# Attention and the w3 product in one block of instructions, and the last stretch's width taken by a branch

## What is computed

```python
attn = softmax(where(block_i >= block_j, q @ k.T / 8, -1e9)) @ v        # 4 x 8 heads, 576 x 64
x = attn, heads side by side                                             # 2304 x 512
h = (x @ w1) * (x @ w2) @ w3 ;  x = h @ w_out                             # w3 1024 x 1024, w_out 1024 x 512
noisy = x @ w_gate + log1p(exp(x @ w_noise)) * noise                      # top 2 of 8, softmax weights
out[t] = sum over its 2 experts of weight * relu(x[t] @ e_w1[e]) @ e_w2[e]
```

## Time and profile before

| | us |
|---|---|
| median of 3 runs | 1051.24 (1050.34 to 1051.44) |
| the profiled execution's own time | 1052.73 |
| its span | 1050.6 |
| PE busy | 1019.5 (97%) |
| DVE, ACT, POOL busy | 443.0, 365.1, 540.7 |

### The profile page before, as it was taken

One profiled execution on the slowest core, in us unless ns is written; L12 is line 12 of the kernel. 1 busy time (PEld: TensorE's weight loads), 2 busy tenths in 40 slices (PEclk: granted clock), 3 DMA queues, 4 the chain that ended last, 5 costly groups with the idle time before them and its releaser, 6 DMA issues.

```text
span 1050.6 us, 16706 instructions
## 1 busy us (share of the span) xinstructions
PE 1019.5 (97%) x5927; PEld 937.4 (89%) x5928; DVE 443.0 (42%) x935; ACT 365.1 (35%) x679; POOL 540.7 (51%) x426
## 2 busy tenths in 40 slices
PE   7999999898999999999999999999999999999996
PEld 5999999787989898989898988889898989898995
DVE  5788888664224243333325742222222223222211
ACT  5999888753212232222223411212121212111110
POOL 8688899530000202020202229968778787878742
PEclk8999999999999999999999999999999999999998
DMA  8788887293970101010402165362717163634303
GB/s 168 169 199 191 202 205 175 69 269 100 369 281 2 60 0 60 0 60 0 140 1 85 48 250 126 92 167 67 192 37 213 20 195 65 190 70 140 41 4 47
DMA packets 73681, 125.25 MB, mean 119 GB/s; under 512 B 13073, under 2 KB 30609, under 8 KB 73634
## 3 DMA queue, kind: packets, MB, share of 16 engines
q1 hardware_dynamic: 64594, 103.74, 34.1%
q0 software_dynamic: 8960, 20.61, 9.9%
...
## 4 chain that ended last, share of the span: by engine, by line
PE 72%; POOL 1%; DVE 1%; issue 1%; ACT 0%; POOLq 0%; DVEq 0%
PE ps_turn L1617 11%; PE ps_b L1593 10%; PE ps_x L1593 10%; PE ps_a L1670 9%; PE ps_x L1688 9%; PE ps_b L1670 9%; PE ps_small L1617 8%; PE ps_a L1573 1%; PE ps_small L1565 1%; PE ps_turn L1555 1%; POOL w_high L1148 1%; POOL w_low L1154 1%; POOL out L1196 0%; PE ps_small L1547 0%; POOLq L892 0%
## 5 line engine op out<-in xcount | busy, mean ns | idle before, releaser
L1139 POOL DMA_INDIRECT expert_rows<-x_rows,slot_idx x36 | 41.7, 1159 | 307.5 <-DVE slot_idx L1493 298.4
L1196 POOL DMA_INDIRECT out<-y_tile,out_rows x40 | 63.3, 1581 | 77.1 <-DVE y_tile L1357 72.4
L1226 ACT CAST xT_high<-ps_a 128x512 fp32r<-128x512 f32 x40 | 23.3, 587 | 197.3 <-PE ps_a L1573 197.3
L1593 PE MATMUL ps_b<-xT_high,w_high 128*128 128x256 f32 (+3 forms) x256 | 78.0, 305 | 2.1 <-DVE xT_low L1341 1.4
L1294 ACT COPY prod<-ps_a 128x384 f32<-128x384 f32 x48 | 23.0, 479 | 163.7 <-PE ps_b L1670 163.7
L1500 DVE TENSOR_TENSOR prod<-ps_b,prod 128x384 f32<-128x384 f32 x48 | 26.7, 557 | 125.5 <-ACT prod L1294 125.5
L1617 PE MATMUL ps_turn<-wo_high,hT_high 128*128 128x512 f32 x192 | 76.2, 397 | 1.4 <-DVE hT_low L1348 1.4
L1593 PE MATMUL ps_x<-xT_high,w_high 128*128 128x256 f32 (+3 forms) x256 | 77.3, 302 | 0.0
L1593 PE MATMUL ps_x<-xT_high,w_low 128*128 128x256 f32 (+3 forms) x256 | 77.2, 302 | 0.0
L1593 PE MATMUL ps_x<-xT_low,w_high 128*128 128x256 f32 (+3 forms) x256 | 77.2, 302 | 0.0
L1593 PE MATMUL ps_b<-xT_high,w_low 128*128 128x256 f32 (+3 forms) x256 | 77.2, 302 | 0.0
...
## 6 DMA issues: line engine op xcount, KB each, us to landing
...
```

Of the source, the lines that this page charges most:

```text
L1139: nc.gpsimd.indirect_dma_start(out=rows_dram, out_offset=bass.IndirectOffsetOnAxis(ap=slot_idx[:, k, t:t + 1], axis=0), in_=x_rows[:, t, : ...
L1196: nc.gpsimd.indirect_dma_start(out=out, out_offset=bass.IndirectOffsetOnAxis(ap=out_rows[:, j:j + 1], axis=0), in_=y_tile[j][:], in_offset ...
L1226: nc.scalar.copy(xT_high[:, :, j * P:(j + 1) * P], ps_xT[j % XS][:].rearrange("p (c t) -> p c t", t=P)).then_inc(xhigh, 1)
L1593: mm = nc.tensor.matmul(ps_hT[q % HS][:, 0:rows.stop - rows.start], lhsT[:, c, f * P:(f + 1) * P], rhs[:, c, rows], start=(n == 0), stop=( ...
```

## The change

It does three things. (1) The two first blocks become one: the w3 product's buffers lie where operands of earlier pairs were (the operands are placed anew for that), its two PSUM tiles are the `work` banks that attention shared for its maxima, and the cuts that PE's first w3 tile needs are written into ACT's and DVE's last attention step. The barrier between the two is gone. (2) The sums, inverses and their spreading for pairs 14 and 15 go through SP's queue instead of POOL's (`settle`, `settle_last`), between the loads of w3 and of w1 and w2; for pair 15 the store and the spread stand behind the first four pieces of w1 and w2 and w3's tiles 1 to 3. (3) The last stretch takes its width by the branch that the others have.

```diff
-def attention(nc, qT, kT, v, identity, rows_q, rows_k, xT, prefetch, prefetched, kept, done):
+def attention_and_fuse(nc, qT, kT, v, identity, rows_q, rows_k, xT, prefetch, prefetched, kept, done, fuse):
...
+        fused = [work[:, SHARED + u] for u in range(2)]
+        cut_out, cut_w3, fuse_on = fuse(ctx, fused, values_done, len(UNITS) * PAIRS, out_taken, normalized, PAIRS)
...
+
+            def settle(n):
+                if n == PAIRS - 1:
+                    gather_sums(n)
+                else:
+                    store_inverses(n)
+                    spread_inverses(n)
+
+            def settle_last():
+                store_inverses(PAIRS - 1)
+                spread_inverses(PAIRS - 1)
+
+            sp.wait_ge(q_rested, 2 * PAIRS)
+            sp.wait_ge(k_rested, 2 * PAIRS)
+            sp.wait_ge(turned_done, after(PAIRS - 2, "late1"))
+            fuse_on["sync"](sp, settle, settle_last)
...
-            for p in range(-2, PAIRS):
+            for p in range(-2, PAIRS + 2):
...
                 each(low, p, "second0")
                 each(low, p, "second1")
+                if p == PAIRS - 1:
+                    invert(p - 1)
+                    cut_w3["low"](0, 0, [0])
                 each(low, p, "late0")
                 if p > -2:
                     each(cast_q, p + 2)
+                if p == PAIRS - 1:
+                    cut_out["low"](0)
                 each(low, p, "late1")
+                if p == PAIRS - 1:
+                    for c in (1, 2):
+                        cut_out["low"](c)
+            fuse_on["vector"](dve, range(3, FUSE_CHUNKS), lambda: invert(PAIRS - 1))
...
                 if p == 0:
                     set_rows(2)
+                if p == PAIRS - 1:
+                    act.wait_ge(prefetched, 16 * sum(len(some) for some in prefetch))
+                    act.wait_ge(q_rested, 2 * PAIRS)
+                    act.wait_ge(k_rested, 2 * PAIRS)
+                    cut_w3["high"](0, 0, [0])
                 each(exps, p, "second0")
                 each(exps, p, "second1")
+                if p == PAIRS - 1:
+                    cut_out["high"](0)
                 each(exps, p, "late0")
                 each(copy_max, p + 1, 0)
+                if p == PAIRS - 1:
+                    cut_out["high"](1)
                 each(exps, p, "late1")
                 each(copy_max, p + 1, 1)
+                if p == PAIRS - 1:
+                    for c in (2, 3):
+                        cut_out["high"](c)
+            fuse_on["scalar"](act, range(4, FUSE_CHUNKS))
...
                 each(values, p, "second0")
                 each(values, p, "second1")
                 each(values, p, "late0")
+            fuse_on["tensor"](pe)
...
-def fuse_output_weights(nc, w1, w2, w3T, parts, raw, prefetched, xT, kept, done, PAIRS):
+def fuse_output_weights(nc, ctx, fused, values_done, VALUES, out_taken, normalized, PAIRS, w1, w2, w3T, parts, raw, chunks):
...
-            load_w3(1, 1)
-            sp.wait_ge(out_low_ready, per)
-            load_in(0, 0, 0)
-            load_w3(2, 0)
-            for k in range(1, PIECES):
-                sp.wait_ge(out_low_ready, per * (k + 1))
-                load_in(k // 2, k % 2, k)
-            with sp.Fori(0, DC // 2 - 1) as a:
-                for k in range(PIECES):
-                    load_w3(PIECES * a + k + 3, (k + 1) % 2)
-                    sp.wait_ge(in_low, PIECES * a + k + 1)
-                    load_in(2 * a + k // 2 + 2, k % 2, k)
...
-            for h in range(2):
-                pool.wait_ge(out_taken[h], PAIRS)
-                nc.gpsimd.dma_start(sums[h * D:(h + 1) * D, (PAIRS - 1) % 2], row_of_sums(tmp, PAIRS - 1, h)).then_inc(last_sums, 16)
-            store(PAIRS - 2)
-            spread(PAIRS - 2)
-            store(PAIRS - 1)
-            normalize(PAIRS - 2)
-            spread(PAIRS - 1)
-            normalize(PAIRS - 1)
...
+        load_w3(1, 1)
+        settle(PAIRS - 2)
+        settle(PAIRS - 1)
+        sp.wait_ge(out_low_ready, per)
+        load_in(0, 0, 0)
+        load_w3(2, 0)
+        for k in range(1, PIECES):
+            sp.wait_ge(out_low_ready, per * (k + 1))
+            load_in(k // 2, k % 2, k)
+
+        def four(a):
+            for k in range(PIECES):
+                load_w3(PIECES * a + k + 3, (k + 1) % 2)
+                if isinstance(a, int) and a == k == 0:
+                    settle_last()
+                sp.wait_ge(in_low, PIECES * a + k + 1)
+                load_in(2 * a + k // 2 + 2, k % 2, k)
+
+        for a in range(DC // 2 - 1):
+            four(a)
...
+        for c in left:
+            if c == half:
+                w3_cut_high(0, 0, [1])
+            out_cut_high(c)
+        w3_cut_high(0, 1)
+        act.wait_ge(values_done, VALUES)
+        act.wait_ge(out_taken[1], PAIRS)
+        act.wait_ge(normalized, 3 * (PAIRS - 2))
...
+            dve.wait_ge(in_high, 2 * m + u + 1)
+            if slot == PIECES - 1:
+                dve.wait_ge(normalized, 3 * PAIRS)
...
+        for c in left:
+            if c == half:
+                w3_cut_low(0, 0, [1])
+            out_cut_low(c)
+        invert_last()
+        w3_cut_low(0, 1)
...
                 pe.wait_ge(weights_cut, 2 * CUTS * before + CUTS)
                 first_product(g, before, 0)
-                if last:
-                    first_product(g, before, 1)
-                else:
-                    step = pe.value_load(widths_i[0:1, bass.ds(g, 1)], min_val=0, max_val=len(WIDTHS) - 1)
-                    for k, width in enumerate(WIDTHS):
-                        with pe.If(step == k):
-                            first_product(g, before, 1, width)
+                step = pe.value_load(widths_i[0:1, bass.ds(g, 1)], min_val=0, max_val=len(WIDTHS) - 1)
+                for k, width in enumerate(WIDTHS):
+                    with pe.If(step == k):
+                        first_product(g, before, 1, width)
                 pe.wait_ge(weights_cut, 2 * CUTS * before + 2 * CUTS)
```

353 lines of the change are left out of this document (170 added, 183 removed).

## The result

The changed kernel took **1045.69 us** (median of 8 runs, 1044.68 to 1049.76) where the kernel before, run beside it, took 1051.58 (8 runs, 1050.34 to 1054.29): a ratio of 0.9948, 95% interval 0.9933 to 0.9964, or 5.5 us less by the ratio. Forecast were 6.7 us less. So it is faster, as forecast, by somewhat less than forecast; the time lies 1.2 us above the 1044.5 of the forecast and inside its range of 1042.4 to 1047.8.

The account below looks back on a forecast made before the run. PE, busy 97% of the span, bounds the kernel. Gains of 4.1 us at the hand-over and 2.56 in the last stretch sum to 6.7, taking the median from 1051.24 to 1044.5; range 1042.4 to 1047.8.

Parts of the forecast that it names:

- Last product: Hand-over: attention's last product (pair 15, `late1`) starts 0.81 us later, at 204.20, behind ACT's three added casts.
- First tile: PE's first w3 tile at the hand-over: follows attention's last product without barrier, clock stays up, ends at 210.7.
- The first rival: Hand-over: the clock falls after all during PE's first w3 tile; 1.6 us given back, 1046.1; chance 8%.
- DVE cuts a 128x512 chunk in 0.61 us: Hand-over: DVE's price per cut, by which its last chunk for the first w3 tile is done by 209.75.
- Second tile: Second w3 tile waits for pair 15's gathered sums, reciprocal and cut; starts at 210.9, not 215.04: 4.1 us gained.
- it only multiplies now: Stage after the hand-over: moving the issues from POOL's queue to SP's costs POOL nothing.
- The stage after it: From the second w3 tile on: SP's load chain and pair 15's normalization keep up; cost 0, range 0 to 2 us.
- slack of 1.2 us: w3's tile 4 behind pair 15's store and spread on SP: first half cut at 226.0, needed at 227.2.
- the moderate SP rival: SP's queue makes tile 3, 4 or 5, or the normalization, late by 1 to 2.5 us: 1046.3; chance 15%.
- Second fall: Lower clock behind the 2.80 us standstill at the w3 product's end, 0.50 in 257 to 259: kept as is.
- The second rival: The clock's second fall, behind the 2.80 us standstill before 256.08, goes away: priced 1.6 us, 1042.9; chance 10%.
- Last stretch: Second part of the last stretch: 320 columns instead of 384, 14.09 us for 16.65, 2.56 us gained; branch costs 0.

Follow-up runs that it names:

- after: First profiled execution of the changed kernel, which has the whole change against the kernel before: it took 1049.76 us; median of the runs 1045.69 us, ratio 0.9948.
- its second profile: The changed kernel measured once more with nothing altered, and profiled again: 1047.49 us (12 runs), ratio 0.9959 to the kernel before.
- the kernel with two pairs on DVE: Changed kernel, but DVE multiplies pairs 14 and 15, pair 13's spread goes one step earlier, tile 4's load ahead of pair 15's spread: 1045.66 us, ratio 0.994.
- the width alone: The kernel before with only the last stretch's width branch added: 1048.56 us (12 runs), ratio 0.9966.
- the quiet kernel: Changed kernel, but POOL multiplies one column instead of all for pairs 13 and 14, so the output is another: 1046.97 us in its one run.

## Why the prediction was right, and where it was off

**Last product.** Forecast 0.81 us later for ACT's three casts; measured 0.90 and 1.33 in the two profiles of the changed kernel, and 0.80 (6.34 against 5.54) in eight of the twelve profiles with the block, among them every one in which POOL was out of the way. In the four others the first cut of `out_low`, ahead of `low` of `late1`, met POOL's pair 13: 1.10 us in after, 1.53 in its second profile, 1.45 and 1.83 in two experiments, and 0.73 to 0.87 in the kernels with this order where the last product was on time. The term was right, the excess is the contention.

**First tile.** No barrier, no gap ahead of the first w3 matmul, clock at 1.00: right. The first rival did not come in the changed kernel, with 0.61 and 1.03 us of standstill ahead of the last product in its two profiles; it came with 1.34 in the kernel with two pairs on DVE. What failed is the step "DVE cuts a 128x512 chunk in 0.61 us". Three of the ten cuts of `out_low` and of the first w3 tile fell to POOL's pair 13 and took 1.0 to 1.2. DVE's next step, `take_out`, started at 209.02, 2.96 us after `low` of `late1`, where the prediction's own steps give 1.83.

**Second tile.** Forecast 6.7 us after the last product, measured 8.26 and 8.27; 6.63 to 6.67 in the four kernels without POOL beside those cuts. The step held that the sums are the last thing that DVE waits for. They landed in time (the reciprocal at 213.36 has no wait), since DVE was late itself, and the tile's own cut then took 1.19 where 0.61 was priced. So the term of 4.1 us came out as 2.5, from the anchor (17.19 before, 14.70 after), and the contention is what it lacked. The size of the term hangs on the execution as well: it is 2.0 with the second profile of the changed kernel, and 3.5 if the hand-over in the profile of the width alone (18.22) stands for before. The sentence on POOL, "it only multiplies now", priced these multiplications at nothing for others; they cost 1.6 us, and 0.1 to 0.5 ahead of the last product.

The Trainium skill has the rule, and I had not weighed it: "SBUF — State Buffer", section "SBUF: two separate sides", says that a DVE instruction with two SBUF inputs and a GpSimd instruction that reads SBUF need the same port pair, which one holds for a whole instruction while the other stands. That ports are the reason is the Trainium skill's word, which no run here can show; the runs agree in kind: cuts with both operands in SBUF double (0.61 to 1.23 each), the one with an operand in PSUM stays at 0.68, and the two engines' undisturbed times add up.

**The stage after it.** Forecast 0 for SP's chain with 0 to 2 in the range; measured 0.18, and this from the slow cuts (second tile to third 5.62 rather than 5.44). The landing of the store was well sized, 6.2 against 6.1. But the "slack of 1.2 us" was not there: with the hand-over as short as I had forecast it, in the quiet kernel, the store took 7.7 us instead of 6.1 and tile 4 was 1.4 us late. Had POOL cost nothing, the moderate SP rival would have been the result, at some 1046 (an estimate: 1051.24 less the 2.7 us that the quiet kernel gains from the anchor to the gated product, less 2.56). Two errors in part covered each other, and that part of the hit is luck.

**Second fall.** Kept as it was, and it stayed in the changed kernel. The second rival was right as a mechanism: in eleven profiles with this gap open (2.8 us, of whichever kernel) the clock fell in ten and not in one, and that one gained 1.55 us, 1.6 in the prediction. So the same standstill costs in one execution and not in another; this case shows it once. That fits what the Trainium skill, "TensorE: Matmul & The Clock Gate", Part 1, says, that the gate's window runs free of the kernel's start. With the gap filled it fell behind it in none of three. The prediction's "both falls that this trace shows" was wrong, though: the trace of before has the clock low from 11 to 21 us too, in the first pairs, and once more at its very end. And 1.6 is not the price of every fall: in one profile each, the one at the hand-over lasted long enough to cost 1.0 more, and the one behind the gap 1.2 more.

**Last stretch.** Forecast 2.56, measured 2.57 by the rows and 3.6 (2.0 to 5.2) by the ratio of the width alone. The branch showed no cost there: right.

**The sum.** 6.7 forecast, 5.2 by the trace from the anchor, 5.5 (3.8 to 7.0) and 4.3 (2.6 to 6.0) by the ratios. The 1.5 that the trace lacks is the contention at the hand-over: 8.0 to 8.3 us with it, 6.65 without. The runs alone would not show it, since the forecast lies inside the first interval.
